# Two small feed-forward layers behind a dynamic convolution: second-layer down products with the gates as stationary operand, results by tokens in four banks

## What is computed

```python
w = softmax(weight_gen, axis=-1)                     # (2, 4096, 8, 7)
x = sum over k of w[..., h, k] * x[s - 6 + k, h]     # (8192, 192)
h = x @ w_in1;  g = np.maximum(0.01 * h, h);  x = g @ w_out1
h = x @ w_in2;  r = np.maximum(h, 0.0);       y = (r * r) @ w_out2
```

## Time and profile before

| | us |
|---|---|
| median of the runs (1121.07 to 1121.29) | 1121.15 |
| span of the profiled execution | 1119.2 |
| median less that span | 1.95 |
| TensorE matmuls busy | 1114.3 (100%) |
| TensorE weight loads busy | 1080.9 (97%) |
| VectorE busy | 874.6 (78%) |
| ScalarE busy | 654.9 (59%) |
| DMA queue 1, share of 16 engines | 11.9% |

### The profile page before, as it was taken

One profiled execution on the slowest core, in us unless ns is written; L12 is line 12 of the kernel. 1 busy time (PEld: TensorE's weight loads), 2 busy tenths in 40 slices (PEclk: granted clock), 3 DMA queues, 4 the chain that ended last, 5 costly groups with the idle time before them and its releaser, 6 DMA issues.

```text
span 1119.2 us, 22845 instructions
## 1 busy us (share of the span) xinstructions
PE 1114.3 (100%) x9906; PEld 1080.9 (97%) x9906; DVE 874.6 (78%) x1053; ACT 654.9 (59%) x785; POOL 8.5 (1%) x15
## 2 busy tenths in 40 slices
PE   9999999999999999999999999999999999999998
PEld 8999999999999999999999999999999999999998
DVE  8998886978769787786977869878697786975575
ACT  6666656565565565646656565564656656566564
POOL 2000000000000000000000000000000000000000
PEclk9999999999999999999999999999999999999999
DMA  5311010200102001020010200102001010000001
GB/s 167 115 43 55 14 56 2 54 17 15 55 1 58 11 16 55 3 58 9 15 55 6 58 8 16 55 8 58 5 15 54 11 55 5 16 15 15 2 1 29
DMA packets 81203, 36.54 MB, mean 33 GB/s; under 512 B 58452, under 2 KB 78674, under 8 KB 81104
## 3 DMA queue, kind: packets, MB, share of 16 engines
q1 hardware_dynamic: 81104, 35.10, 11.9%
HBM read 23.25 MB, written 6.29 MB: 26 GB/s over the span
## 4 chain that ended last, share of the span: by engine, by line
PE 99%; DVE 0%; DMA 0%; ACT 0%; issue 0%; ACTq 0%; DVEq 0%
PE h_pair L1149 46%; PE y_main_psum L1195 31%; PE y_rest_psum L1199 21%; PE h_pair L1158 0%; PE h_pair L1094 0%; DMA tap_logits<-in_weight_gen_dram 0%; PE y_main_psum L1094 0%; DVE tap_product L730 0%; PE y_rest_psum L1223 0%; PE h_pair L1244 0%; DVE x_windows L965 0%; ACT x_windows L595 0%; DVE tap_sum L710 0%; DVE h_pair L716 0%; DVE tap_shifted L704 0%
## 5 line engine op out<-in xcount | busy, mean ns | idle before, releaser
L1149 PE MATMUL h_pair<-x_parts,w_in_parts 64*128 64x512 f32 x4590 | 563.5, 386 | 0.0
L1149 PEld LDWEIGHTS h_pair<-x_parts,w_in_parts 64*128 64x128 f32 x4590 | 505.6, 184 | 14.7 <-DVE w_in_parts L682 0.2
L1195 PE MATMUL y_main_psum<-g_hi,w_out_parts 64*128 64x512 f32 x2040 | 431.1, 386 | 0.0
L919 DVE TENSOR_TENSOR g_lo<-g,g_hi 128x1024 fp32r<-128x1024 f32 x255 | 311.1, 1220 | 122.6 <-ACT g_hi L581 96.0
L569 ACT ACTIVATE g_hi<-h_pair 128x1024 fp32r<-128x1024 f32 x125 | 128.5, 1028 | 193.4 <-PE h_pair L1149 193.3
L581 ACT ACTIVATE g_hi<-g 128x1024 fp32r<-128x1024 f32 x127 | 134.7, 1061 | 170.5 <-DVE g L910 170.5
L1195 PEld LDWEIGHTS y_main_psum<-g_hi,w_out_parts 64*128 64x128 f32 x2040 | 224.9, 184 | 6.5 <-issue 0.2
L1199 PE MATMUL y_rest_psum<-g_lo,w_out_parts 64*128 64x512 f32 x1020 | 215.5, 386 | 0.0
L1199 PE MATMUL y_rest_psum<-g_hi,w_out_parts 64*128 64x512 f32 x1020 | 215.5, 386 | 0.0
L1195 PE MATMUL y_main_psum<-g_lo,w_out_parts 64*128 64x512 f32 x1020 | 215.5, 386 | 0.0
L910 DVE SCALAR_TENSOR_TENSOR g<-h_pair,u 128x1024 f32<-128x1024 f32 x127 | 155.2, 1222 | 37.9 <-ACT u L575 36.1
(11 more groups left out here) (123 smaller groups left out, 429.8 us busy)
## 6 DMA issues: line engine op xcount, KB each, us to landing
x_windows<-in_x_dram SPq DMA_DIRECT2D x12, 960.0 KB
out_dram<-raw_w_in SPq DMA_DIRECT2D x360, 16.0 KB, 1.5
raw_w_in<-tap_product SPq DMA_DIRECT2D x336, 16.0 KB, 1.8
raw_w_out<-in_moe_w_out_dram SPq DMA_DIRECT2D x16, 192.0 KB, 3.9
tap_logits<-in_weight_gen_dram SPq DMA_DIRECT2D x16, 112.0 KB, 2.9
raw_w_in<-in_moe_w_in_dram SPq DMA_DIRECT2D x8, 192.0 KB, 3.6
raw_w_in<-in_moe_w_in_dram SPq DMA_DIRECT2D x8, 128.0 KB, 3.2
x_windows<-in_x_dram SPq DMA_DIRECT2D x2, 384.0 KB, 4.4
```

The costliest lines, as they stand in the source:

```text
L919: dve.tensor_tensor(GL[n % 4][:, :, :], gate[n % 2][:, :, :], GH[n % 4][:, :, :].bitcast(fp32), ALU.subtract).then_inc(glo_ready, 1)
L1149: last = pe.matmul(h[:, i, :], w[r, slot, a, c], v[r, slot, b, :], start=first, stop=end)
L1195: return pe.matmul(ym[rows][:, :], w[r, c], g[r, i, :], start=start, stop=stop)
```

## The change

All 128 second-layer down steps, the last ones included, get a new form, `down_by_tokens`. The gates are now stationary (64 inner features x 128 tokens) and the weights move: 384 columns (all parts) against the gates' high part, 192 (high part) against their low part. A result is 128 tokens x 384 in one PSUM bank: the sum of the high-part products in the first 192 columns, the low weights' products behind them. The four blocks of 128 tokens have a bank each. A visit is one half's four matmuls on one bank (two tiles of inner features, two parts). The halves go through the banks in turn, half 0 in the order 0, 2, 1, 3 and half 1 two visits on; a half waits, from its third visit of a chunk on, for the other to have left the bank (`lower_left`, `upper_left`). Both halves add up in the same banks, and the first two visits of each clear them. `fold` for the second layer is then: ScalarE copies the low weights' columns (two banks at a time), VectorE adds them to the first 192 columns straight into the rows to be stored. No transpositions are left there, `last_down`, `last_turn` and `last_fold` go, and a chunk is stored with four transfers of 96 KB with runs of 768 bytes. The last step's low gates are waited for whole. First-layer downs, ups and the convolution keep their form; their four banks are the same four under new names.

```diff
+        def down_by_tokens(s, j):
+            n = s * PR + j
+            left = (lower_left, upper_left)
+            pe.wait_ge(glo_ready, n + 1 if n < SEGS * PR - 1 else n + 2)
...
+            if j == 0:
+                banks_free(s)
+            for v in range(4 * j, 4 * (j + 1)):
+                for i in range(2):
+                    for g, width in ((GH[n % 4], 2 * D), (GL[n % 4], D)):
+                        for half, r in enumerate(ROWS):
+                            q = BANK_ORDER[(v + 2 * half) % 4]
+                            if v > 1 and i == 0 and width > D:
+                                pe.wait_ge(left[1 - half], VISITS * CHUNK[s] + v - 1)
+                            done = pe.matmul(y_banks[:, q, 0:width], g[r, i, q * P:(q + 1) * P], WO[1][r, j + i * PR, 0:width],
+                                             start=v < 2 and i == 0 and width > D, stop=v >= VISITS - 2 and i == 1 and width == D)
+                            if i == 1 and width == D:
+                                done.then_inc(left[half], 1)
...
         # ScalarE, fold(s) of the second layer
+                if LAYER[s] == 1:
+                    for pair in range(2):
+                        act.wait_ge(lower_left, finished(CHUNK[s], pair))
+                        act.wait_ge(upper_left, finished(CHUNK[s], pair))
+                        act.activation(low_of(pair), y_banks[:, 2 * pair:2 * pair + 2, D:2 * D], ACT.Copy).then_inc(low_parts, 1)
...
         # VectorE, fold(s) of the second layer
+                    for pair, summed in enumerate((y_first_out, y_last_out)):
+                        dve.wait_ge(low_parts, 2 * c + pair + 1)
+                        rows, banks = y_tok[:, 2 * pair:2 * pair + 2, :], y_banks[:, 2 * pair:2 * pair + 2, :]
+                        dve.tensor_tensor(rows[:, :, 0:P], banks[:, :, 0:P], low_of(pair)[:, :, D - P:D], ALU.add)
+                        dve.tensor_tensor(rows[:, :, P:D], banks[:, :, P:D], low_of(pair)[:, :, 0:D - P], ALU.add).then_inc(summed, 1)
...
         # SyncE, store(c)
-                for q in range(P // BL):
-                    for g in range(P // BL):
-                        sync.dma_start(bass.AP(out.tensor, first + g * BL * TPP * D + q * BL, [[TPP * D, BL], [D, TPC], [1, BL]]),
...
+                for pair, summed in enumerate((y_first_out, y_last_out)):
+                    sync.wait_ge(summed, c + 1)
+                    for q in range(2 * pair, 2 * pair + 2):
...
+                        sync.dma_start(to, y_tok[:, q, :]).then_inc(stored, 16)
```

More of the change, by code:

```diff
@@ L276, in conv_two_ffn_kernel, with finished, low_of @@
         y_taken = sem("y_taken")
-        y_turned = sem("y_blocks_transposed")
-        last_main_turned = sem("last_y_main_transposed")
         turned_taken = sem("transposed_pair_taken")
[L281 to L300, removed]
+        lower_left = sem("lower_rows_left_bank")
+        upper_left = sem("upper_rows_left_bank")
+        low_parts = sem("y_low_parts_copied")
+        y_first_out = sem("y_first_rows_summed")
+        y_last_out = sem("y_last_rows_summed")
+        VISITS = 4 * PR
+        BANK_ORDER = (0, 2, 1, 3)
+        def finished(c, pair):
+            return VISITS * (c + 1) - 1 + pair
+        def low_of(pair):
+            return folds[:, 2 * NC + pair * 2 * D:2 * NC + (pair + 1) * 2 * D].rearrange("p (q d) -> p q d", q=2)
         block = ctx.enter_context(nc.Block())
@@ L436, in _ @@
                     move(c + 2)
[L437 to L441, removed]
+                store(c)
+            sync.wait_ge(stored, STORED * NCH)
         @block.gpsimd
@@ L991, in segment @@
                         fold(s - 1)
-                    if s and j == 2:
+                    if s and LAYER[s - 1] == 0 and j == 2:
                         fold_end(s - 1)
-                    if s and LAYER[s - 1] == 1 and j == 3:
-                        blocks(CHUNK[s - 1], s - 1)
                     if s == 1:
@@ L1212, in down @@
                 last.then_inc(down_done, 1)
-            def last_down():
-                n = SEGS * PR - 1
-                gh, gl = GH[n % 4], GL[n % 4]
-                for i in range(2):
-                    w = WO[1][:, PR - 1 + i * PR, :]
-                    pe.wait_ge(glo_ready, n + 1 + i)
-                    for g in (gh, gl):
-                        for rows, r in enumerate(ROWS):
-                            last = pe.matmul(yr[rows][:, :], w[r, P:2 * P], g[r, i, :], start=False, stop=i == 1 and g is gl)
-                last.then_inc(last_rest_done, 1)
-                for i in range(2):
-                    w = WO[1][:, PR - 1 + i * PR, :]
-                    for c, g in ((2 * P, gh), (0, gh), (0, gl)):
-                        for rows, r in enumerate(ROWS):
-                            last = pe.matmul(ym[rows][:, :], w[r, c:c + P], g[r, i, :], start=False, stop=i == 1 and g is gl)
-                last.then_inc(down_done, 1)
@@ L1259, in _, with down_of @@
+            def down_of(s, j):
+                if LAYER[s] == 1:
+                    down_by_tokens(s, j)
+                else:
+                    down(s, j)
             turn_first()
```

165 lines of the change are left out of this document (46 added, 119 removed).

## The result

The changed kernel takes **1126.92 us** (median of five, 1126.81 to 1127.04) against 1121.15 us before: +5.8 us, a ratio of 1.0052 with a 95% interval of 1.0040 to 1.0064. Its profiled span is 1125.1 us, 5.9 above the 1119.2 of before, and both parts of the difference can be read from it.

A forecast was written before the change was run, and what follows sets the result against it. TensorE's matmul stream was taken to bound the kernel. The span of 1119.2 plus 7.2 us for the down steps less 0.3 at the end gave 1126.1, and 1.95 from span to median gave 1128.0 us, range 1117 to 1139.

The forecast's parts named there:

- TensorE alone counts: Whole kernel: only TensorE's own stream and the program's end matter; savings on VectorE or in stores are worth nothing by themselves.
- A 384 pair at 173.3 ns: High-gate pairs of second-layer downs: 160 ns of columns plus 13.3 ns taken as fixed per pair.
- A 192 pair at 117 ns: Low-gate pairs of second-layer downs: the next gates' load sets the spacing, 113 to 127 ns; step +56 ns; chance 0.66.
- rival 2: Second-layer down steps: a load counts 108 to 112 ns, step -5 to +2, total 1116 to 1123 us; chance 0.12.
- the sum: Total over 128 second-layer down steps and the end: +7.2 us in TensorE's stream, -0.3 us at the end.
- The waits for the other half cost nothing: Visits' first loads in second-layer downs: 580 ns available against some 0.34 us needed, so no cost.
- The end, -0.3 us: Behind the last matmul: copies, adds and four stores take 4.0 to 4.6 us against 4.65 before.
- 1, the hidden load: Every 192-column pair: the load is hidden and 93.3 ns bind, step -133 ns, total 1103.8 us; chance 0.17.
- Rival 3: Turns of the banks between halves: late signals stall TensorE, total over 1170 us; chance 0.05.

The follow-up runs named there:

- low_256: Changed kernel with 256 instead of 192 moving columns in the low gates' matmuls of every second-layer down: 1134.17 us, ratio 1.0116.
- all_384: Changed kernel with 384 moving columns for the low gates too, so no pair is short; single run: 1196.07 us.
- low_128: Changed kernel with 128 instead of 192 moving columns in the low gates' matmuls: 1130.42 us, ratio 1.0083.
- narrow_96: Changed kernel with every stationary gate block cut from 128 to 96 tokens, moving columns unchanged: 1110.99 us, ratio 0.9911.
- turn_after_one: Changed kernel with the halves one visit apart in the ring of four banks, so half 0 waits for the visit just issued; single run: 1265.71 us.
- low_first: Changed kernel with the low gates' pair ahead of the high gates' pair in all but a chunk's first two visits: 1126.60 us, ratio 1.0050.
- last_chunk_only: Kernel before with the new down steps in the last segment alone, one final store, last eight ups reading reordered tokens: 1121.11 us, ratio 0.9999.
- last_chunk_staged: Kernel before with new last-segment downs and one final store, tokens reordered while the input is copied, ups reading in a row: 1120.52 us, ratio 0.9996.

## Why the prediction was right, and by what luck

The time was forecast as 1128.0 us in a range of 1117 to 1139, slower with a chance of 0.66. It is 1126.9. Step by step:

- **TensorE alone counts**: right: nothing waits at L1165, and the 41 us less of VectorE and the twenty stores less a chunk brought nothing.
- **A 384 pair at 173.3 ns, the overhead fixed per pair**: right in kind. `low_256` fits it to the nanosecond (293.3); in `all_384` the pairs stand 173 ns apart once a step has settled, 175 on average.
- **A 192 pair at 117 ns**: the mechanism is shown by `low_256`, `low_128` and `narrow_96`; the size was off. 284.6 ns for both pairs less 173.3 leaves **111.3 ns**. That is outside the 113 to 127 on which the forecast's chance of 0.66 stood, and inside rival 2's 108 to 112. The dry load of the earlier trace rows had said 110 to 113; I had moved up towards, where the load follows transpositions. Its 120 to 127 ns did not come back in a stream of one kind. With 111.3 the step is 8 x 284.6 = 2277 ns, +10 and not +56.
- **Not in the sum**: a down step changes the up behind it. By the starts in the trace most steps take 4327 ns with their up, against 2277 + 2040: 10 more. The up behind the two adjacent steps of each chunk takes 27 more still. The stream's cost is then 0.18 us a chunk, +2.9 us, where the sum had +7.2; of these 2.9 the load explains 128 x 10 ns = 1.3 us, and the other 1.6 have no cause that a run shows.
- **The waits for the other half cost nothing**: right, shown by the empty waits and by what `turn_after_one` costs, 0.33 us a wait.
- **The end, -0.3 us**: wrong, +2.9. The sentence that failed is that each issue takes 0.35 and the landing 2.3 us "or, being a quarter as large, somewhat sooner". The last store was issued at +2.5 and not +1.9, since each issue took 0.54, and its last packet ended 4.3 us behind that. The landing is what counted: a pattern with four tokens outermost kept the transfers on four DMA engines, and their packets ran without a break for 4.9 us (1119.53 to 1124.39), whenever the later ones were issued. The adds, at +1.27, had been placed well (+1.5). Had I read the changed store's `[[D, TPC], [TPP * D, BL], [1, D]]` for the order of its dimensions, the end would have been open up to 8 us.
- **Rivals**: 1, the hidden load, fell. The 81 ns cited there from the Trainium skill (TensorE: Matmul & The Clock Gate, section "Back-to-back issue gap") do not hold for this stream either: behind these short matmuls it is 111. Rival 2, the marginal case, is what happened in the stream, not the forecast: its upper end, 8 x (173.3 + 112), +2 us, is within 1 us of the measured +2.9. Alone, with the end as I had it, the time would have been 1123.7, barely slower. Rival 3 fell: no wait stands at L1165, and one visit less of distance costs 0.33 us a wait (`turn_after_one`).

So two misses of opposite sign, -4.2 us in the stream and +3.2 at the end, hid each other in the total, and 1126.9 came so near to 1128.0 by luck.

## What to carry to other kernels

Swapping the stationary and the moving operand is not priced by columns alone: a matmul shorter than its successor's load (here 128 columns, 111 ns from one start to the next, against 226.7 for a 512-column pair) costs the load, so ten long pairs beat sixteen with half of them short, though these have a tenth less columns (by 3 us in 1121, of which less than half is the load's). And a store is priced by its pattern's outermost dimension before its bytes or its runs: 128 rows outermost used two thirds of the DMA engines' time, four tokens outermost a quarter, and at the end of this program that is 3 to 4 us that nothing covers.

## What the hardware showed that was not expected

- A down step with 128-column low pairs is slower than with 192 (1130.4 against 1126.9 us): its two pairs take 286.4 ns for 284.6, and the up behind it is slower too.
- Behind steps whose pairs are short or have 384 columns the ups are slower than the 2.04 us that they take behind 512-column pairs, also where no pair is short and no load is late. A step with its up takes more than its own pairs' distances and 2.04 us add up to: 0.01 us in most steps of the changed kernel, 0.03 in `low_128`, some 0.07 in `narrow_96` and `all_384`, and nothing in `low_256`, whose ups are back at 2.04. The cause stays open; `low_first` excludes only the order inside a visit.
- A moving operand read in runs of 32 elements costs 6.7 ns more per 512-column pair, 233.3 against 226.7 (`last_chunk_only`; read in a row again, the time is 0.6 us less, `last_chunk_staged`).
- A load of 128 columns takes 0.11 us at the upper clock level and 0.16 at the lower one, while 32 columns fewer save 26 ns at the upper. One fixed part and one part that scales with the clock do not explain both: the first two figures give the scaling part some 0.05 us at the upper level, a quarter of which is 13 ns and not 26.
